# Fused attention and two expert layers: VectorE's attention order written by steps, one product moved to GpSimd

## The reference

```python
q_pool = q.reshape(B, H, S // 2, 2, D).mean(axis=3)              # 576 queries
scores = scale * np.matmul(q_pool, k.transpose(0, 1, 3, 2))      # 576 x 1152
scores = scores - np.max(scores, axis=-1, keepdims=True)
attn = np.exp(scores)
attn = attn / (np.sum(attn, axis=-1, keepdims=True) + 1e-09)
x = np.matmul(attn, v)                                           # 576 x 64 per head
h = x @ w_in;  g = h * tanh(softplus(h));  y = g @ w_out         # layer 0, 1152 tokens, 512 -> 2048 -> 512
h = y @ w_in2; g = elu(h);                 out = g @ w_out2      # layer 1
```

## Time and profile before

| | us |
|---|---|
| median of 3 runs | 676.5 (676.04 to 676.55) |
| the profiled execution | 676.52 |
| its span in the profile | 674.7 |
| attention stage, first score matmul to the last values | about 17 to 268 |
| TensorE busy | 657.4 |
| GpSimd, VectorE, ScalarE busy | 418.4, 412.8, 390.9 |

### The profile page before, as it was taken

One profiled execution on the slowest core, in us unless ns is written; L12 is line 12 of the kernel. 1 busy time (PEld: TensorE's weight loads), 2 busy tenths in 40 slices (PEclk: granted clock), 3 DMA queues, 4 the chain that ended last, 5 costly groups with the idle time before them and its releaser, 6 DMA issues.

```text
span 674.7 us, 12472 instructions
## 1 busy us (share of the span) xinstructions
PE 657.4 (97%) x4042; PEld 641.8 (95%) x4042; DVE 412.8 (61%) x708; ACT 390.9 (58%) x733; POOL 418.4 (62%) x384
## 2 busy tenths in 40 slices
PE   8899999999999999999999999999999999999998
PEld 7899899999999999999999999999999999999998
DVE  7788878788888862777776666777553232223222
ACT  5788888888888788655565555555633222222220
POOL 5678696979797866677776775777554422222221
PEclk9999999999999999999999999999999999999999
DMA  7666666665655421132200001222123010001001
GB/s 202 174 169 178 177 170 178 176 180 169 190 164 161 131 70 50 40 84 63 63 30 0 0 4 44 65 62 63 63 67 89 19 47 0 0 0 47 1 1 48
DMA packets 35857, 57.94 MB, mean 86 GB/s; under 512 B 7568, under 2 KB 13024, under 8 KB 35808
## 3 DMA queue, kind: packets, MB, share of 16 engines
q1 hardware_dynamic: 35488, 57.02, 29.9%
q10 hardware_dynamic: 320, 0.30, 0.2%
HBM read 33.29 MB, written 2.40 MB: 53 GB/s over the span
## 4 chain that ended last, share of the span: by engine, by line
PE 61%; POOL 11%; DVE 10%; issue 9%; ACT 7%; DMA 1%; SPq 1%; POOLq 0%; ACTq 0%; DVEq 0%
PE py L584 7%; PE py L585 6%; PE py L586 6%; PE pH L570 6%; PE pH L569 6%; PE pH L571 6%; PE ps L501 4%; PE po L517 4%; PE ps L502 4%; PE po L518 4%; PE pm L487 4%; PE po L519 4%; POOL fg L1101 4%; POOL gl L1086 3%; DVE pl L857 3%
## 5 line engine op out<-in xcount | busy, mean ns | idle before, releaser
L1086 POOL TENSOR_TENSOR gl<-fg,gh 128x384 fp32r<-128x384 f32 x96 | 98.0, 1021 | 134.8 <-ACT gh L763 132.6
L837 DVE TENSOR_REDUCE part_max<-pm 128x1 f32<-128x384 f32 x225 | 117.9, 550 | 31.6 <-PE pm L487 29.2
L584 PE MATMUL py<-gh,wout_h 128*128 128x384 f32 x384 | 129.1, 336 | 2.2 <-DVE xl L942 1.1
L585 PE MATMUL py<-gl,wout_h 128*128 128x384 f32 x384 | 128.3, 334 | 0.0
L1029 POOL TENSOR_TENSOR pl<-p,ph 128x576 fp32r<-128x576 f32 x72 | 105.5, 1470 | 36.8 <-ACT p L675 35.6
L586 PE MATMUL py<-gh,wout_l 128*128 128x384 f32 x384 | 128.3, 334 | 0.0
L571 PE MATMUL pH<-xh,win_l 128*128 (+1 forms) x384 | 128.3, 334 | 0.0
L570 PE MATMUL pH<-xl,win_h 128*128 (+1 forms) x384 | 128.3, 334 | 0.0
L569 PE MATMUL pH<-xh,win_h 128*128 (+1 forms) x384 | 128.3, 334 | 0.0
L669 ACT ACTIVATE ph<-ps 128x576 fp32r<-128x576 f32 x144 | 93.7, 651 | 37.5 <-PE ps L502 34.3
L921 DVE RECIPROCAL fi<-fp 128x192 f32<-128x192 f32 x48 | 64.9, 1353 | 52.4 <-POOL fp L1094 52.4
(11 more groups left out here) (79 smaller groups left out, 1359.1 us busy)
## 6 DMA issues: line engine op xcount, KB each, us to landing
kh<-k_hi SPq DMA_DIRECT2D x60, 144.0 KB, 3.2
w_raw<-w_in SPq DMA_DIRECT2D x32, 256.0 KB, 3.0
w_raw<-w_out SPq DMA_DIRECT2D x32, 256.0 KB, 2.7
q_raw<-qT SPq DMA_DIRECT2D x16, 288.0 KB, 3.1
k_pack<-kP SPq DMA_DIRECT2D x16, 288.0 KB, 3.2
v_raw<-v SPq DMA_DIRECT2D x16, 288.0 KB, 3.4
kl<-k_pack SPq DMA_DIRECT2D x32, 144.0 KB, 2.4
q<-q SPq DMA_DIRECT2D x16, 144.0 KB, 2.5
```

The source lines that it names most:

```text
L584: pe.matmul(out, hi, gh[:, f % 4, :], start=(f == 0), stop=False)
L585: pe.matmul(out, hi, gl[:, f % 4, :], start=False, stop=False)
L837: dve.tensor_reduce(part_max[:, par, j:j + 1], pm[:, at % 2, 0:MC], AX.X, ALU.max).then_inc(m_read, 1)
L1086: pool.tensor_tensor(gl[:, f % 4, :], fg[:, f % 2, :], gh[:, f % 4, :].bitcast(F32), ALU.subtract).then_inc(gl_ready, 1)
```

## The change

VectorE's attention part is no longer a loop over chunks with tiles behind them, but a loop over TensorE's steps: for each step it handles that step's early and late chunks, and the subtraction of the tile kt+3 stands before, between or behind them as `SPLIT_PLACE` says (0, 1, 2). The counts of chunks in each step are new, with tables of their own for heads 0, 1 and 2. In even heads tile 8 moves from GpSimd to VectorE. In odd heads tile 0 moves from VectorE to GpSimd and tile 3 from GpSimd to VectorE: GpSimd's tiles are now (1, 3, 5, 7) and (0, 1, 5, 7). `finalize` becomes `multiply_x` on GpSimd, in step 2 of the odd heads (and, for the last pair, in layer 0). `sum_few` has a second entry of 1e-9 that is set once, and the addition is a reduction over the two. In `pv` and `max_chunk` the waits stand in another order. Other tasks of GpSimd and ScalarE have new steps.

```diff
--- before.py
+++ after.py
@@ -13,25 +13,23 @@
 
 AHEAD = 3
 
-POOL_KT = ((1, 3, 5, 7, 8), (1, 3, 5, 7))
+POOL_KT = ((1, 3, 5, 7), (0, 1, 5, 7))
 
 PREP = 3
 
 
 WARM_FIRST, WARM_ROW, WARM_SCORES = 20, 28, 2
 FIRST_ORDER = ((0, 3), (1, 2), (4, 5), (6, 7), (8, 9), (10, 11), (12, 13), (14,))
-EARLY_CHUNKS = (2, 3)
-FIRST_CHUNKS = ((3, 1), (1, 2), (1, 1), (1, 0), (1, 0), (2, 1), (1, 1), (1, 1), (1, 1))
-CHUNKS = ((1, 0), (2, 0), (2, 0), (0, 0), (2, 0), (1, 1), (2, 0), (1, 1), (1, 1))
-
-
-FIRST_SPLIT_BEHIND = {2: (1, 0), 6: (1, 2), 11: (1, 4), 14: (1, 6)}
-SPLIT_BEHIND = {3: (2, 8), 5: (1, 0), 8: (1, 2), 12: (1, 4), 14: (1, 6)}
-INVERT_BEHIND, FINALIZE_BEHIND = 3, 13
-
-
-GPSIMD_AT = {'split_k': (0, 0), 'sum_q': (3, 2), 'split_v': (3, 1), 'split_q': (8, 4), 'split_w': (5, 7), 'split_x': (0, None)}
-SCALAR_AT = {'split_v': (0, 0), 'split_w': (1, 2), 'round_k': (3, 5), 'split_q': (7, 6), 'split_x': (None, 7)}
+EARLY_CHUNKS = (3, 3)
+EARLY_SPLIT = 1
+FIRST_CHUNKS = (((2, 0), (3, 1), (2, 2), (0, 0), (1, 1), (0, 1), (1, 1), (1, 1), (1, 1)), ((1, 0), (2, 0), (2, 0), (1, 0), (2, 0), (2, 1), (1, 0), (1, 0), (2, 1)), ((1, 0), (2, 1), (0, 1), (0, 0), (1, 0), (2, 1), (1, 0), (1, 0), (2, 1)))
+CHUNKS = ((1, 0), (2, 0), (1, 1), (0, 1), (0, 1), (2, 1), (1, 0), (1, 0), (2, 1))
+SPLIT_PLACE = (2, 1, 0, 1, 2, 1, 1, 2, 2)
+INVERT_AT = 4
+
+
+GPSIMD_AT = {'multiply_x': (None, 2), 'split_k': (1, 1), 'sum_q': (2, 2), 'split_v': (2, 2), 'split_q': (5, 4), 'split_w': (5, 8), 'split_x': (0, None)}
+SCALAR_AT = {'split_v': (0, 2), 'split_w': (5, 0), 'round_k': (3, 5), 'split_q': (5, 6), 'split_x': (None, 6)}
 
 
 def wait(eng, sem, value):
@@ -98,7 +96,8 @@
 
             o_rows = sa("o_rows", [P, 3, SQ])
             x_pair = sa("x_pair", [P, SQ])
-            sum_few = sa("sum_few", [P, FEW])
+            sum_few = sa("sum_few", [P, 2, FEW])
+            sum_all = sa("sum_all", [P, FEW])
             inv_few = sa("inv_few", [P, FEW])
 
             vt = [sa(f"vt{i}", [P, KT, 4, D], F32R) for i in range(2)]
@@ -148,7 +147,7 @@
         kh_spread, kl_done, vh_done, vl_done = sem("kh_spread"), sem("kl_done"), sem("vh_done"), sem("vl_done")
         m_filled, m_read, max_ready = sem("m_filled"), sem("m_read"), sem("max_ready")
         first_filled, first_read = sem("first_filled"), sem("first_read")
-        warm_set, first_half = sem("warm_set"), sem("first_half")
+        warm_set, first_half, preset_least = sem("warm_set"), sem("first_half"), sem("preset_least")
         s_filled, s_read = sem("s_filled"), sem("s_read")
         pl_vec, pl_pool = sem("pl_vec"), sem("pl_pool")
         pv_done, o_copied = sem("pv_done"), sem("o_copied")
@@ -231,13 +230,16 @@
         def score_ap(n, kt):
             return score_bank(n, kt)[:, :, 0:HQ]
 
+        def step_chunks(n):
+            return FIRST_CHUNKS[n] if n < len(FIRST_CHUNKS) else CHUNKS
+
         def chunks_at(n, kt, late):
 
-            counts = FIRST_CHUNKS if n == 0 else CHUNKS
-            begun = sum(map(sum, counts[:kt])) + (counts[kt][0] if late else 0)
-            begun += sum(EARLY_CHUNKS) if n == 0 else sum(EARLY_CHUNKS) + sum(map(sum, FIRST_CHUNKS)) - NCH
+            counts = step_chunks(n)
+            begun = sum(EARLY_CHUNKS) + sum(sum(map(sum, step_chunks(h))) for h in range(n))
+            begun += sum(map(sum, counts[:kt])) + (counts[kt][0] if late else 0)
             for c in range(begun, begun + counts[kt][late]):
-                head = n + 1 + c // NCH
+                head = 1 + c // NCH
                 if head < HEADS:
                     yield head, c % NCH
 
@@ -365,7 +367,7 @@
                 sp.wait_ge(o_copied, m + 1)
                 wait(sp, sum_kept, pair)
                 source = D * (1 - par)
-                sp.dma_start(sum_few[par * D:par * D + D, :],
+                sp.dma_start(sum_few[par * D:par * D + D, 0, :],
                              o_rows[source:source + 1, o_slot(m), :].rearrange("o (r c) -> o r c", c=FEW)).then_inc(sums_in[par], 16)
 
             def move_o(p):
@@ -480,10 +482,10 @@
             def max_chunk(n, j):
 
                 at, (t, c) = chunk_count(n, j), divmod(j, 3)
+                wait(pe, m_read, at - 1)
                 if j == 0:
                     pe.wait_ge(kh_spread, 64 * (n + 1))
                     pe.wait_ge(q1_spread, 64 * (n + 1))
-                wait(pe, m_read, at - 1)
                 pe.matmul(pm[:, at % 2, 0:MC], q1[:, n % 3, t * P:t * P + P], kh[n % 3][:, c * MC:c * MC + MC],
                           start=True, stop=True).then_inc(m_filled, 1)
 
@@ -505,10 +507,9 @@
             def pv(n, kt):
                 par, slot = n % 2, n % 4
                 if kt == 0:
+                    wait(pe, o_copied, n)
                     wait(pe, vh_done, n + 1)
                     wait(pe, vl_done, n + 1)
-
-                    wait(pe, o_copied, n)
                 wait_pl(pe, n, kt, par)
                 v_one = vt[par][:, kt, 0:2, :].rearrange("p a d -> p (a d)")
                 v_low = vt[par][:, kt, 2:4, :].rearrange("p a d -> p (a d)")
@@ -861,20 +862,19 @@
 
                 dve.wait_ge(sums_in[0], 16 * (p + 1))
                 dve.wait_ge(sums_in[1], 16 * (p + 1))
-                dve.tensor_scalar(sum_few[:, :], sum_few[:, :], 1e-9, None, ALU.add).then_inc(sum_kept, 1)
+                if p == 0:
+                    dve.wait_ge(preset_least, 1)
+                wait(dve, sum_inv, p)
+                dve.tensor_reduce(sum_all[:, :], sum_few[:, :, :].rearrange("p a f -> p f a"), AX.X,
+                                  ALU.add).then_inc(sum_kept, 1)
                 dve.wait_ge(sum_kept, p + 1)
                 wait(dve, inv_in, 16 * p)
-                dve.reciprocal(inv_few[:, :], sum_few[:, :]).then_inc(sum_inv, 1)
-
-            def finalize(p):
-                dve.wait_ge(inv_spread, 32 * (p + 1))
-                dve.wait_ge(o_moved, 16 * (p + 1))
-                dve.tensor_tensor(x_pair[:, :], o_rows[:, o_slot(2 * p), :], x_pair[:, :], ALU.mult).then_inc(x_ready, 1)
-
+                dve.reciprocal(inv_few[:, :], sum_all[:, :]).then_inc(sum_inv, 1)
 
             dve.memset(ph[:, 0, 0:HQ].bitcast(F32), 1.0).then_inc(warm_set, 1)
             dve.memset(q1[:, :, SQ:QP].bitcast(F32), 0.0).then_inc(preset_pad, 1)
             dve.memset(row_max[:, :, :].bitcast(F32), 0.0).then_inc(preset_row, 1)
+            dve.memset(sum_few[:, 1, :], 1e-9).then_inc(preset_least, 1)
             dve.memset(kl[0][D:2 * D, :].bitcast(F32), 0.0).then_inc(kl_preset[0], 1)
             dve.memset(q2[0][D:2 * D, :].bitcast(F32), 0.0).then_inc(q2_preset[0], 1)
             dve.wait_ge(q_in, 16)
@@ -892,18 +892,31 @@
                 first_group(g)
             dve.wait_ge(first_read, NG)
             turn_row(0)
-            for m in range(1, HEADS + 2):
-                for j in range(NCH):
-                    if m < HEADS:
-                        max_chunk(m, j)
-                    if j == INVERT_BEHIND and m % 2 == 0 and 4 <= m <= HEADS:
-                        invert((m - 4) // 2)
-                    if j == FINALIZE_BEHIND and m % 2 == 0 and 4 <= m <= HEADS:
-                        finalize((m - 4) // 2)
-                    if j in (SPLIT_BEHIND if m > 1 else FIRST_SPLIT_BEHIND):
-                        back, kt = (SPLIT_BEHIND if m > 1 else FIRST_SPLIT_BEHIND)[j]
-                        if 0 <= m - back < HEADS and kt in VKT[(m - back) % 2]:
-                            split_p(m - back, kt)
+            def split_ahead(n, kt):
+                nxt = ahead(n, kt)
+                if nxt is not None and nxt[1] in VKT[nxt[0] % 2]:
+                    split_p(*nxt)
+
+            for j in range(EARLY_CHUNKS[0] + EARLY_SPLIT):
+                max_chunk(1, j)
+            split_p(0, 0)
+            for j in range(EARLY_CHUNKS[0] + EARLY_SPLIT, sum(EARLY_CHUNKS)):
+                max_chunk(1, j)
+            split_p(0, 2)
+            for n in range(HEADS):
+                for kt in range(KT):
+                    if SPLIT_PLACE[kt] == 0:
+                        split_ahead(n, kt)
+                    for head, j in chunks_at(n, kt, 0):
+                        max_chunk(head, j)
+                    if SPLIT_PLACE[kt] == 1:
+                        split_ahead(n, kt)
+                    for head, j in chunks_at(n, kt, 1):
+                        max_chunk(head, j)
+                    if SPLIT_PLACE[kt] == 2:
+                        split_ahead(n, kt)
+                    if kt == INVERT_AT and n % 2 == 0 and n > 0:
+                        invert(n // 2 - 1)
 
             attention_over(dve)
 
@@ -988,8 +1001,6 @@
                     if base == 0:
                         for f in range(4):
                             unit_step(layer, t, f, 4 + f, 1)
-                            if f == 0:
-                                finalize(PAIRS - 1)
                         division_over(dve)
                     with dve.Fori(1 if base else 2, 4) as i:
                         for f in range(4):
```

(10 more changed lines are left out.)

## The result

The changed kernel takes 667.15 us (median; 666.94 to 667.87) against 676.48 for the kernel before: a ratio of 0.9865, 95% interval 0.9848 to 0.9882, or 9.3 us less. The prediction was 671.4, and its whole range with the rivals was 667.5 to 676.8. The profiled execution spans 665.4 us.

A forecast was written before the change was run, and what follows sets the result against it. The prediction took TensorE's stalls between matmuls, at `pv(n,0)` and in odd heads at tile 8's scores, as the bound. Its terms -6.2 - 1.4 + 1.8 + 0.4 + 0.3 = -5.1 took 676.5 to 671.4 us; range with rivals 667.5 to 676.8.

The forecast's parts named there:

- What bounds the kernel: TensorE's starts: a pair of heads loses 2.6 us that no busy share shows, some 20 us over the attention stage.
- The product leaves VectorE: Odd heads, step 2: without the product the stall at tile 8's scores goes, 6 x 1.03 = -6.2 us.
- The product on GpSimd: Odd heads, step 2: it takes 1.43 us on GpSimd and is hidden by 0.4 us.
- The addition: Even heads, step 4: as a reduction 0.35 us less on VectorE, gaining nothing in itself; bounds 0 and -2 us.
- The new step orders: Step 8's extra early chunk shrinks the stall at `pv(n,0)` by 0.2 us in 7 odd heads, not even ones: -1.4 us.
- Tiles moved: VectorE's subtractions go from 9 to 10 per pair, 0.76 us, covered: cost 0.
- The order of waits: `pv(n,0)`: with `o_copied` first, two more satisfied waits follow the copy, 0.06 us each in 15 heads: +1.8 us.
- The third rival: Waits cost nothing and the chunks' stalls shrink too (even heads' halved, -2 us): 667 to 669 us; chance 15%.
- Start: Three early chunks delay head 0's first scores by 0.63 us, partly regained: between -0.5 and +1, taken as +0.4 us.
- Layer 0: The last product delays GpSimd by 0.46 us where it feeds TensorE: between 0 and +1.4, taken as +0.3 us.

The follow-up runs named there:

- e3: The kernel before with only the pair's product moved to GpSimd, step 2 of odd heads: 671.52 us, ratio 0.9929.
- e2: The kernel before with only the new order of waits in `pv(n,0)`: 674.69 us, ratio 0.9976.
- e6: The changed kernel with the product back on VectorE, behind the row's work at the end of step 2: 676.24 us, ratio 0.9997.
- e4: The changed kernel with the product back on VectorE, between the early and late chunks of step 2 of odd heads: 666.45 us, ratio 0.9853.
- e5: The kernel before with the product still on VectorE but three steps later, behind chunk 3 of the next row (step 5): 672.50 us, ratio 0.9941.
- e12: The changed kernel with 1e-9 added by a `tensor_scalar` as before, not by a reduction: 667.20 us, ratio 0.9861.
- e8: The changed kernel with one chunk of heads 3 and up moved back from step 8 to step 7: 668.22 us, ratio 0.9877.
- e1: The changed kernel with the old order of waits in `pv(n,0)`, `o_copied` written third instead of first: 669.48 us, ratio 0.9897.
- e10: The changed kernel with the old division of tiles between GpSimd and VectorE: 668.43 us, ratio 0.9880.
- e7: The changed kernel with `o_copied` written second instead of first among the waits of `pv(n,0)`: 667.19 us.
- e9: The kernel before with both the product on GpSimd and the new order of waits: 668.75 us, ratio 0.9884.

## Why the prediction was right or wrong

**What bounds the kernel.** Right: TensorE's starts and not its busy share showed what was to be had, and the change lives in heads 3 to 14 (-9.24 of -9.3 us).

**The product leaves VectorE.** The size in the old order was right (-6.2 forecast; 1.03 six times in e3, -4.9 with what layer 0 gives back). The reading was half wrong. It took 1.77 us as the product's price; that was its price beside GpSimd, and alone it is 0.75, and the difference is mostly time in which it waits for a GpSimd instruction that was there first (e2, e6). The minimum was in the prediction and used only for GpSimd's side. e4, e5 and e6 show that place and collision decide, not the engine: on VectorE in the new order it costs nothing (666.45) or everything (676.24). So this is a step whose reason failed although its size fitted: with the new order the stall is gone even with the product on VectorE (e4), and that the sum came near for this term is in part luck.

**The product on GpSimd.** Right: 1.43 us, hidden, the queue as worked out. (The row's work in that reckoning is 139.94 - 138.86 = 1.08 us and not 1.05, which changes nothing.) The Trainium skill (GPSIMD Engine Reference, section Key points) says that GpSimd contends for the SBUF interfaces with VectorE instructions that have two SBUF inputs, and the runs agree both ways: 1.87 us for the product and 1.30 instead of 0.81 for GpSimd's sum when they meet (e6), 0.75 for the product when they hardly do or don't (e4, e5).

**The addition.** Right: nothing (e12).

**The new step orders.** The chunk in step 8 was right as a mechanism and about right in size (-1.4 forecast, -1.1 by e8). The split between heads was wrong: it was to bring 0.2 us into odd heads and nothing into even ones. In e1, which has the new step order with the old waits, `pv(n,0)` is late by 0.24 us in odd and 0.26 in even heads, against 0.37 in both before.

**Tiles moved.** Forecast 0, measured -1.3 (e10), at the end of attention and in the entry to layer 0 and not in the heads with chunks. In the entry they matter only because the product is on GpSimd.

**The order of waits. This is the step that failed.** The prediction put it as "after the copy the queue still has two more satisfied waits to pass", +1.8 us. The price was about right, 0.05 to 0.07 us per satisfied wait (e7, e1), but the sign was wrong, and the bounds of 0 to 6.3 us had no room for a gain: the program passes them in another order than the source writes them, and the new order takes three waits from behind the copy. Measured: -1.7 us alone (e2), -2.3 in the changed kernel (e1). From +1.8 to -2.3 are 4.1 us, and the prediction missed by 4.25. That these are so near is in part chance: the tiles (-1.3 against 0) and the smaller misses of the other terms nearly cancel. In hindsight the trace had a hint: if only `pl` had stood behind the copy, one wait would have cost 0.21, four times what e7 shows.

**The third rival.** Its 667 to 669 came nearest, but not by its reasons. It had the waits at nothing, where they bring 2.3 us, and 2 us from smaller stalls of the chunks in even heads, where all stalls other than those of `pv(n,0)` and of scores shrank by 0.5 in heads 3 to 14.

**Start and layer 0.** Start: +0.4 forecast. Head 0 ends 1.33 later, and by the end of head 2 that is made up (-0.11 in sum), but this contains the gain of the waits. Against e9, which has the product on GpSimd and the new waits with the old tables, the changed kernel is 0.2 us later at the end of head 2. Layer 0: +0.3 forecast, +0.29 measured, and 0.4 against e4.

## What to carry to other kernels

Before pricing an instruction that is to be moved, look at its minimum, and at what the other engines do while it takes longer; here the product on VectorE waited for whatever GpSimd had begun before it. Another place in the same queue can be worth nearly as much as another engine, and one place later can cost everything. Where an engine stands at a matmul with several waits, look in the compiled program at which one is passed last, and let that be the one that comes last in time. Parts of such a change don't simply add up: a gain reaches the end only if the next stall in line doesn't take it back.
